# Routing logits of an attention stage: two 64-token halves as one 128-column stationary operand

## What is computed

```python
# attention, a linear recurrence: B=4, H=8, S=768, D=48
for t in range(S):
    y[:, :, t] = r_t @ (state + u * outer(k_t, v_t))
    state = w * state + outer(k_t, v_t)
x = y.transpose(0, 2, 1, 3).reshape(3072, 384)
# mixture of experts
do_compute = x @ w_skip > 0
logits = xc @ w_gate            # 8 experts
e_idx = argmax(logits); gate_w = softmax(logits)[e_idx]
out = x; out[do_compute] += gate_w * (relu(xc @ w1[e]) @ w2[e])
# gated layers
h = (x @ w1) * (x @ w2) @ w3
return h @ w_out
```

## Time and profile before

| | |
|---|---|
| time, three runs | 615.3, 614.32, 615.23 us (median 615.23) |
| profiled execution, first to last instruction | 612.5 us |
| PE busy | 595.1 us, 97% of the span |
| DVE, ACT, POOL busy | 286.4, 228.1, 156.5 us |
| attention stage, until PE's last L337 record | 121.3 us from the span's start |

### The profile page before, as it was taken

How to read it: one execution, slowest core, us unless ns; L and a number is a source line. 1 busy time by engine, 2 the same in 40 slices (tenths; PEclk the granted TensorE clock), 3 DMA queues, 4 the chain that set the end, 5 groups by cost and what they waited for, 6 DMA issues and landing times.

```text
span 612.5 us, 17307 instructions
## 1 busy us (share of the span) xinstructions
PE 595.1 (97%) x7355; PEld 532.3 (87%) x7355; DVE 286.4 (47%) x459; ACT 228.1 (37%) x410; POOL 156.5 (26%) x179
## 2 busy tenths in 40 slices
PE   6699999999999999999999999999999999999997
PEld 6699999766999999999688888888898888888886
DVE  5489889283777777774121332232132133223212
ACT  3156666444665555552321222132132122213212
POOL 7568887215055544441230000000000000000000
PEclk9899999999999999999999999999999999999999
DMA  7779997596566777630400030020011001001001
GB/s 130 133 145 187 188 184 188 206 313 241 181 237 246 277 274 271 237 130 20 164 1 0 1 103 1 1 103 1 0 57 48 1 1 51 1 1 51 1 0 52
DMA packets 104258, 67.80 MB, mean 111 GB/s; under 512 B 79708, under 2 KB 98272, under 8 KB 104216
## 3 DMA queue, kind: packets, MB, share of 16 engines
q1 hardware_dynamic: 76360, 57.91, 30.8%
q10 hardware_dynamic: 25552, 4.72, 4.1%
q0 software_dynamic: 2304, 4.59, 2.3%
HBM read 55.92 MB, written 12.20 MB: 111 GB/s over the span
## 4 chain that ended last, share of the span: by engine, by line
PE 50%; DVE 0%; ACT 0%; issue 0%
PE gl_pab L1508 32%; PE gl_po L1523 8%; PE p_pair L1523 8%; PE gl_pab L1496 1%; PE p_pair L93 0%; DVE gl_g_lo L1590 0%; DVE gl_g_sb L1588 0%; ACT gl_g_hi L1568 0%; ACT gl_a_sb L1565 0%; DVE gl_o_sb L1601 0%
## 5 line engine op out<-in xcount | busy, mean ns | idle before, releaser
L1588 DVE TENSOR_TENSOR gl_g_sb<-gl_a_sb,gl_pab 128x512 f32<-128x512 f32 x48 | 33.0, 688 | 186.3 <-ACT gl_a_sb L1565 186.3
L1508 PE MATMUL gl_pab<-gl_xT_hi,wm_lo 128*128 128x512 f32 x288 | 112.9, 392 | 0.0
L1508 PE MATMUL gl_pab<-gl_xT_lo,wm_hi 128*128 128x512 f32 x288 | 112.8, 392 | 0.0
L1508 PE MATMUL gl_pab<-gl_xT_hi,wm_hi 128*128 128x512 f32 x288 | 112.1, 389 | 0.0
L1565 ACT ACTIVATE gl_a_sb<-gl_pab 128x512 f32<-128x512 f32 x48 | 28.8, 599 | 183.9 <-PE gl_pab L1508 183.9
L1508 PEld LDWEIGHTS gl_pab<-gl_xT_hi,wm_lo 128*128 128x128 f32 x288 | 54.0, 188 | 11.4
L1508 PEld LDWEIGHTS gl_pab<-gl_xT_hi,wm_hi 128*128 128x128 f32 x288 | 54.1, 188 | 10.6 <-DVE gl_xT_lo L1595 0.3
L1508 PEld LDWEIGHTS gl_pab<-gl_xT_lo,wm_hi 128*128 128x128 f32 x288 | 54.0, 188 | 10.5
L1265 PE MATMUL ex_ph<-ex_xT_hi,ew_w_hi 128*128 128x224 f32 x192 | 52.9, 275 | 0.0
L1265 PE MATMUL ex_ph<-ex_xT_hi,ew_w_lo 128*128 128x224 f32 x192 | 52.7, 274 | 0.0
L1265 PE MATMUL ex_ph<-ex_xT_lo,ew_w_hi 128*128 128x224 f32 x192 | 52.7, 274 | 0.0
(11 more groups left out here) (197 smaller groups left out, 1223.3 us busy)
## 6 DMA issues: line engine op xcount, KB each, us to landing
w_in<-in_moe_w SPq DMA_DIRECT2D x8, 1536.0 KB
ew_w_in<-in_moe_w SPq DMA_DIRECT2D x8, 1536.0 KB
w_in<-in_moe_w SPq DMA_DIRECT2D x14, 512.0 KB, 9.4
k_in<-in_k SPq DMA_DIRECT2D x48, 96.0 KB
v_in<-in_v ACTq DMA_DIRECT2D x48, 96.0 KB, 3.5
r_in<-in_r SPq DMA_DIRECT2D x48, 96.0 KB
w_in<-xbuf SPq DMA_DIRECT2D x12, 384.0 KB, 4.1
out<-gl_o_sb SPq DMA_DIRECT2D x12, 384.0 KB, 2.4
```

What stands on the lines that cost most here:

```text
L1508: m = pe.matmul(p_ab[f % 2][w][:, :], a[:, w * KD + k, cols], b[t.slot][:, k, :], start=(k == 0 and n == 0), stop=(k == KD - 1 and n == 2))
L1588: dve.tensor_tensor(g_sb[f % 2][:, :], a_sb[f % 2][:, :], p_ab[f % 2][1][:, :], ALU.mult).then_inc(s_g, 1)
```

## The change

The layout of `xT` goes from (jj, q, token) to (q, jj, token), so that the 128 tokens of a tile lie side by side for each feature block. `logits` then loads all 128 as one stationary operand and makes one matmul for both halves: six matmuls a tile instead of twelve, each with 128 columns loaded where 64 were. Every tile's result goes to the same places of PSUM. ACT's copy writes the new layout, and one zeroing copy is reworded.

```diff
-        xT = [sb(f"xT{i}", [P, 2, KC, C]) for i in range(2)]
+        xT = [sb(f"xT{i}", [P, KC, 2, C]) for i in range(2)]
...
                 for q in range(KC):
-                    for jj in range(2):
-                        for rg in range(2):
-                            i = pe.matmul(p_Y[half(jj), rg, HALF + t.slot * NL:HALF + (t.slot + 1) * NL], xT[t.pr][half(rg), jj, q, :], w_gates[half(rg), q, :],
-                                          start=(q == 0), stop=(q == KC - 1), skip_group_check=True)
+                    for rg in range(2):
+                        i = pe.matmul(p_Y[:, rg, HALF + t.slot * NL:HALF + (t.slot + 1) * NL], xT[t.pr][half(rg), q, :, :].rearrange("p j c -> p (j c)"), w_gates[half(rg), q, :],
+                                      start=(q == 0), stop=(q == KC - 1), skip_group_check=True)
...
-                act.activation(xT[t.pr][:, :, :, :].rearrange("p j q c -> p j (q c)"), p_K[:, :, HALF:HALF + KC * C], ACT.Copy).then_inc(s_xT, 1)
+                act.activation(xT[t.pr][:, :, :, :].rearrange("p q j c -> p j q c"), p_K[:, :, HALF:HALF + KC * C].rearrange("p j (q c) -> p j q c", q=KC), ACT.Copy).then_inc(s_xT, 1)
```

More of the change, by code:

```diff
@@ L470, in _ @@
             for x in xT:
-                zero(x[:, :, :, :].rearrange("p j q c -> p (j q c)"))
+                zero(x[:, :, :, :].rearrange("p q j c -> p (q j c)"))
             zero(A_m[1][:, :, :, :].rearrange("p r m c -> p (r m c)"))
```

## The result

The changed kernel takes 619.08 us (median of 18 runs) against 615.79 us (18 runs of the kernel before beside it): ratio 1.0055, 95% interval 1.004 to 1.0069, so 3.4 us slower by the ratio (3.3 by the medians). Measured a second time it was 619.98 against 615.06 us, ratio 1.0071 (1.0046 to 1.0095), 4.4 us by the ratio (4.9 by the medians). The forecast was 619.1 us, 3.9 more than before.

What follows compares the result with a forecast made beforehand. PE was taken as the bound, with DVE setting one loop tile in four. Terms of 1.1, 0.5, 0, 1.3 and 1.0 us summed to 3.9 us, 615.2 + 3.9 = 619.1 us; 8-in-10 range 614.8 to 623.0.

Steps and rivals of the forecast that it cites:

- The load's price: Logits on PE: 128-column loads cost 0.11 us a pair at the plain matmuls' rate; +0.27 us a tile in sum.
- The first rival: New logits loads run at the transposes' 62 ns a pair, array work unchanged; 615.2 or 614 us; chance 0.08, cured 0.04.
- The second: Rival: logits' pace is set by instructions, so 12 records take 0.18 us; 611.5 us; chance 0.06.
- The third: Rival: load and matmul don't overlap, late issue stays; +0.27 in 23 tiles, 621.9 us upper bound; no separate chance.
- late issue: PE's sequencer issues instructions too late in three of four loop tiles, 0.15 to 0.25 us each; expected mostly to go.
- The copy and the layout at nothing: ACT's xT copy, between 485 ns and twice that, costs nothing because ACT sits idle 0.75 us a tile.
- The four groups behind the loop: Logits groups after the loop, where PE never idles, pass the added cost on whole: 4 x 0.27 = 1.1 us.
- The last two tiles: Final two tiles of the loop run bare, so the added cost shows whole: 0.5 us.
- Five tiles that DVE sets: Loop tiles ending with a 0.33 to 0.48 us wait for k_dec; the added 0.27 disappears in it: 0.
- The others: Thirteen other loop tiles: added cost mostly offset by less late issue; 0.1 us each, 1.3 us in all.
- The first tiles: First four tiles: 1.1 us, up to 1.6 at half clock, some going into waits; taken as 1.0 us.
- The moved stalls: First-pass issue stalls of 2.1 and 2.3 us could fall elsewhere, shifting any case up to 2 us; no separate chance.

Runs made afterwards that it cites:

- twice_96: Changed kernel with an added idle set of six logits matmuls ahead, loading 96 of the 128 columns; 631.22 us, ratio 1.0256 to the kernel before.
- cols48_before: Kernel before, with the updates' matmuls loading 48 columns of k_dec instead of 64; ratio 0.9998 to the kernel before.
- layout_only: Changed kernel's new xT layout, but with the old twelve logits matmuls of 64 loaded columns; 614.95 us against 614.88 before, ratio 0.9999.
- tail_only: Six new logits matmuls only in the four groups behind the loop, old twelve inside, new layout throughout; 615.48 us against 614.94 before, ratio 1.0015.
- twice_128: Changed kernel with its six logits matmuls made twice, 128 columns loaded each time; 634.21 us, ratio 1.0323 to the kernel before.
- k128: Kernel before's 64 loaded columns, but six logits matmuls contracting over all 128 rows, new layout; 616.4 us against 615.06 before, ratio 1.0018.
- actscale_after: Changed kernel with the scaling of the second pair's states moved from POOL to ACT; 620.32 us, ratio 1.007 to the kernel before.
- cols48_after: Changed kernel with the updates' matmuls loading 48 columns of k_dec instead of 64; 618.43 us, ratio 1.0061 to the kernel before.

## Why the prediction was right, step by step

**The load's price: right.** The plain rows and not the transposes' decide: 188 ns a load, 0.11 us a pair, +0.26 us in the bare tile (forecast +0.27). Shown by twice_96 too, which measures 0.83 ns a column in this shape. The first rival (62 ns a pair) is out. The second (a price per instruction) is out by twice_96 and by cols48_before. The third had late issue stay whole, +0.27 us in each tile that PE sets; +0.17 was measured.

**The copy and the layout at nothing: right**, shown by layout_only.

**The four groups behind the loop, 1.1 us: a little too high.** 0.9 us by tail_only and by the timeline: the first group costs 0.28 us, the last two, which stand together, 0.63, and the second nothing, since the weights' product behind it starts 1.01 us after `YT`'s transposes with either form. I had read "PE never idles" as "PE's array is the bound everywhere", and there it is not. Before and after:

```profile
112.86 0.41 PE L292 MATMUL p_R<-ident,YT 64*128 64x64 f32 x8
...
113.87 2.85 PE L93 MATMUL p_pair<-wo,w3T 128*128 128x384 f32 x8
```

```profile
114.70 0.41 PE L292 MATMUL p_R<-ident,YT 64*128 64x64 f32 x8
...
115.71 2.85 PE L93 MATMUL p_pair<-wo,w3T 128*128 128x384 f32 x8
```

**The last two tiles, 0.5 us: right** (2 x 0.26).

**Five tiles that DVE sets, 0 us: wrong.** They did not stay at 4.0 us, they got shorter: 3.82 on average over the four in the steady passes. I took DVE's chain as fixed because it ran without a gap. Its last member was 1.13 us long because POOL's `v_bonus` ran beside it. Shown: `k_decay` is 0.55 everywhere once POOL's work is earlier. That PE's slower pass moved the two apart in the changed kernel is read from its shorter 0.83 us, not tried by itself.

**The others, +0.1 us each: too low.** Over the four steady passes they went from 3.66 to 3.83 on average, +0.17 each. I expected the late issue to go nearly whole. They stand 0.10 us over the bare 3.72; before, they stood 0.20 over the bare 3.46. So half of it went. With the logits at 1.39 us (twice_128) nearly all of it is gone (0.02 left). The cause, that the sequencer lacks a lead, fits twice_128 and k128 but was not isolated: neither a kernel with fewer semaphore instructions on PE was tried, nor what else tells the loop's last two tiles from the others.

These two errors cancel, and that is luck: the 16 steady tiles take 102.79 - 41.58 = 61.2 us instead of 101.75 - 41.87 = 59.9, 1.3 us more (12 x 0.17 - 4 x 0.18), where my terms for them come to 12 x 0.1 = 1.2. In the second profile of the change it is 60.8 us, 0.95 more.

**The first tiles, 1.0 us: a term that isn't a constant.** Up to the first steady tile the first profile of the change is 0.3 us shorter than before's (41.58 against 41.87), the second 2.9 us longer (44.78). That could also be why the changed kernel's runs spread from 616.5 to 622.3 us while those of before spread from 613.7 to 617.5; only the profiled runs show where their time went. Steady tiles, last two tiles and the groups behind the loop make 1.3 + 0.5 + 0.9 = 2.7 us of the 3.4 to 4.4 measured. The rest, 0.7 to 1.7 us, is a remainder: mostly the first 42 us by these profiles, but the second also has 0.7 us behind the loop, and k128 lost 5.7 us there. That it comes from where the half-clock stretches fall is argued from four profiles of kernels with the new logits (the change twice, actscale_after, cols48_after), three of which have one from 34 to 42 us, and not shown by an experiment; why they fall later here stays open. My 1.0 us was worked out from the array's added work, less what waits take up. The moved stalls stood among the rivals, with up to 2 us either way, and two profiles of one and the same kernel lie 3.2 us apart here.

So the price of the new matmuls was right and shown. That the total came out within a microsecond also took luck: two wrong terms that cancel, and a term for the first tiles that the two profiles put at -0.3 and +2.9 us.

## What to carry to other kernels

With few columns moved, a matmul costs its load, and the load goes by the columns loaded: merging two loads of 64 into one of 128 halves the instructions and wins nothing on the array, and it loses when four pieces that loaded at once become two. Take the price of a load from a matmul of the same kind; a transpose in the very same shape loads at twice the rate. And an engine that runs without a gap isn't a fixed bound when one of its operations is stretched by a neighbour.

## What was not expected of the hardware

- A plain float32 load costs 0.81 to 0.84 ns a column at full clock (188 ns for 128 columns, 161 or 162 for 96, 135 for 64) in the shapes 128*128, 64*128, 64*96 and 64*64, and is hidden under nothing when nine columns are moved; a transpose's load 0.42 ns. The Trainium skill, "TensorE: Matmul & The Clock Gate", section "LDWEIGHTS", gives columns divided by 1.2 GHz: the plain loads agree, the transposes' do not.
- A loop body of 1,456 matmul and load records (twice_128) ran without stalls marked issue after 42 us; one of 1,648 had 25.7 us of them there, and the kernel took 60 us more, of which 8 to 10 were expected from its added matmuls.
- Running beside POOL's two-operand work, DVE's `k_decay`, which reads two operands from SBUF, goes from 0.55 us to as much as 1.21 us. `x_out` (L583), which reads one of its two from PSUM, keeps 0.55 us beside `v_bonus` (start 81.32 us, `v_bonus` from 80.86 to 81.69).
